# A transpose pair inside a stream of long matmuls is taken apart: one transpose before the last accumulation step, one behind it

## The reference

```
rel = pos[:, None] - pos[None, :]
mask = (rel >= 0) & (rel < 64)
attn = softmax(where(mask, q @ k.T / 8, -1e9))
x = (attn @ v), heads side by side: 2304 x 512
h = x @ w_in      # 512 x 2048
x = max(0.01 * h, h) @ w_out
h = x @ w_in2
out = (h * cos(h)) @ w_out2
```

## Time and profile before

| | |
|---|---|
| median of three runs | 912.01 us (910.81 to 912.53) |
| span of the profiled execution | 910.0 us, from the first to the last instruction |
| own time of that execution | not recorded beside its span; the median of the runs is 2.0 us above the span |
| mean granted clock of TensorE | 1.000 |
| TensorE matmuls busy | 891.0 us, 98% |
| VectorE, ScalarE, GpSimd busy | 477.5, 393.2, 83.9 us |

### The profile page before, as it was taken

How to read it: one execution, slowest core, us unless ns; L and a number is a source line. 1 busy time by engine, 2 the same in 40 slices (tenths; PEclk the granted TensorE clock), 3 DMA queues, 4 the chain that set the end, 5 groups by cost and what they waited for, 6 DMA issues and landing times.

```text
span 910.0 us, 14462 instructions
## 1 busy us (share of the span) xinstructions
PE 891.0 (98%) x5040; PEld 846.9 (93%) x5040; DVE 477.5 (52%) x1146; ACT 393.2 (43%) x978; POOL 83.9 (9%) x68
## 2 busy tenths in 40 slices
PE   6799999999999999999999999999999999999998
PEld 5799999999999999999999889998999999999997
DVE  6755555545555554555323555545545545545543
ACT  5566444433433343434345534434433434434433
POOL 2254300000000000000256400000000000000000
PEclk9999999999999999999999999999999999999999
DMA  8455322222221222220444300100200100100100
GB/s 279 136 168 177 113 77 64 64 84 63 63 71 64 76 63 73 60 67 0 142 116 139 116 1 0 69 0 0 69 0 0 69 0 0 69 0 0 36 1 36
DMA packets 36878, 59.72 MB, mean 66 GB/s; under 512 B 3952, under 2 KB 24816, under 8 KB 36848
## 3 DMA queue, kind: packets, MB, share of 16 engines
q1 hardware_dynamic: 36848, 59.33, 21.0%
HBM read 49.87 MB, written 9.44 MB: 65 GB/s over the span
## 4 chain that ended last, share of the span: by engine, by line
PE 94%; DVE 3%; ACT 1%; issue 1%; DMA 0%; SPq 0%; ACTq 0%; DVEq 0%
PE h_ps L305 43%; PE y_ps L330 22%; PE y_ps L337 21%; PE s_ps L265 3%; PE t_ps L292 3%; PE t_ps L280 1%; DVE probs L564 1%; DVE x_raw L577 1%; DMA qk_sb<-qk 0%; DVE probs L539 0%; DVE neg_max L546 0%; DVE row_sum L552 0%; ACT w_hi L400 0%; DVE act_in L598 0%; DVE probs L596 0%
## 5 line engine op out<-in xcount | busy, mean ns | idle before, releaser
L305 PE MATMUL h_ps<-x_hi,w_hi 128*128 128x384 f32 x768 | 264.0, 344 | 1.1 <-DVE g_raw L604 0.6
L305 PE MATMUL h_ps<-x_lo,w_hi 128*128 128x384 f32 x768 | 258.3, 336 | 0.0
L305 PE MATMUL h_ps<-x_hi,w_lo 128*128 128x384 f32 x768 | 257.6, 335 | 0.0
L305 PEld LDWEIGHTS h_ps<-x_hi,w_hi 128*128 128x128 f32 x768 | 144.7, 188 | 5.9 <-DVE g_raw L604 1.0
L305 PEld LDWEIGHTS h_ps<-x_hi,w_lo 128*128 128x128 f32 x768 | 144.5, 188 | 3.7
L305 PEld LDWEIGHTS h_ps<-x_lo,w_hi 128*128 128x128 f32 x768 | 144.2, 188 | 0.3 <-DVE x_lo L583 0.3
L610 DVE TENSOR_TENSOR g_lo<-g_raw,g_hi 128x384 fp32r<-128x384 f32 x192 | 107.2, 558 | 68.4 <-ACT g_hi L448 68.4
L448 ACT ACTIVATE g_hi<-g_raw 128x384 fp32r<-128x384 f32 x192 | 100.7, 524 | 93.9 <-DVE g_raw L604 56.1
L589 DVE TENSOR_TENSOR g_raw<-h_ps,act_in 128x384 f32<-128x384 f32 x96 | 53.5, 557 | 164.4 <-ACT act_in L430 164.4
L330 PE MATMUL y_ps<-g_hi,w_hi 128*128 128x384 f32 x384 | 134.1, 349 | 0.0
L430 ACT ACTIVATE act_in<-h_ps 128x384 f32<-128x384 f32 x96 | 47.1, 490 | 194.4 <-PE h_ps L305 194.4
(11 more groups left out here) (43 smaller groups left out, 961.0 us busy)
## 6 DMA issues: line engine op xcount, KB each, us to landing
qk_sb<-qk SPq DMA_DIRECT2D x72, 224.0 KB, 2.6
v_sb<-values SPq DMA_DIRECT2D x72, 128.0 KB, 2.1
w_raw<-w_in SPq DMA_DIRECT2D x32, 256.0 KB, 2.7
w_raw<-w_out SPq DMA_DIRECT2D x32, 256.0 KB, 2.9
layer_out<-y_out SPq DMA_DIRECT2D x6, 768.0 KB, 3.8
x_raw<-layer_out SPq DMA_DIRECT2D x6, 768.0 KB, 5.2
out<-y_out SPq DMA_DIRECT2D x5, 768.0 KB, 4.0
mask_sb<-mask SPq DMA_DIRECT2D x18, 128.0 KB, 2.1
```

Of the source, the lines that this page charges most:

```text
L305: mm = pe.matmul(h_ps[j % 2][:, 0:CH], w[:, j, cols], x[:, kt, :], start=kt == 0 and a == 0, stop=kt == KT - 1 and a == 2)
```

## The change

`transposes` becomes `transpose_half`, called once for each of its two blocks. The waits stay with the first half, the signal `transposed` with the second. In a tile with attention, `up` now stops ahead of its last `up_part` (kt 3); the first transpose is issued, then the three matmuls of kt 3, then the second transpose, then `down`. The loop for the first 12 units calls both halves one after the other, as before. Layer 2 and the last chunk of layer 1 have no attention, and their order is what it was.

```
+            def transpose_half(c, p, banks, a):
+
+                if a == 0:
+                    if p == 0 and banks is first_banks:
+                        pe.wait_ge(ident_in, 16)
+                    pe.wait_ge(probs_done, UNITS * c + p + 1)
+                    if banks is later_banks:
+                        pe.wait_ge(o_copied, UNITS * c + p)
+                    elif p >= 2:
+                        pe.wait_ge(probsT_done, p - 1)
+                t = banks[1][p % len(banks[1])]
+                mm = pe.transpose(t[:, P * a:P * a + P], probs[:, p % PRING, P * a:P * a + P], ident_sb[:])
+                if a == 1:
+                    mm.then_inc(transposed, 1)
+
             def transposes(c, p, banks):
...
                 for a in range(2):
-                    mm = pe.transpose(t[:, P * a:P * a + P], probs[:, p % PRING, P * a:P * a + P], ident_sb[:])
-                mm.then_inc(transposed, 1)
+                    transpose_half(c, p, banks, a)
...
-            def up(n, j):
-
-                pe.wait_ge(g_raw_done, FT * n + j - 1)
-                for kt in range(KT):
+            def up(n, j, kts=range(KT)):
+
+                if kts[0] == 0:
+                    pe.wait_ge(g_raw_done, FT * n + j - 1)
+                for kt in kts:
                     up_part(n, j, kt)
...
-                        up(*ahead)
+                        up(*ahead, range(KT - 1))
                     if attends and 1 <= j <= UNITS:
-                        transposes(n + 1, j - 1, later_banks)
+                        transpose_half(n + 1, j - 1, later_banks, 0)
+                    if not (last and j + LEAD >= FT):
+                        up(*ahead, range(KT - 1, KT))
+                    if attends and 1 <= j <= UNITS:
+                        transpose_half(n + 1, j - 1, later_banks, 1)
                     if not late:
                         down(n, j, layer)
```

More of the change, by code:

```diff
@@ L267, in scores @@
                 mm.then_inc(scores_done, 1)
-            def transposes(c, p, banks):
[L271 to L278, removed]
+            def transpose_half(c, p, banks, a):
[11 more added lines that the diff above has]
+                    mm.then_inc(transposed, 1)
+            def transposes(c, p, banks):
                 for a in range(2):
-                    mm = pe.transpose(t[:, P * a:P * a + P], probs[:, p % PRING, P * a:P * a + P], ident_sb[:])
-                mm.then_inc(transposed, 1)
+                    transpose_half(c, p, banks, a)
             def values(c, p, banks):
```

## The result

The changed kernel takes 914.03 us (median of 13 runs, 912.0 to 915.09) against 912.53 us for the kernel before (13 runs, 910.81 to 913.63): ratio 1.0018, 95% interval 1.0011 to 1.0026, that is 1.6 us more (1.0 to 2.4). The forecast was 913.9 us and 1.9 us more. That the 914.03 lies so close to 913.9 is partly luck: the kernel before came out at 912.53 in these runs and not at the 912.01 from which the forecast counted.

What follows compares the result with a forecast made beforehand. The prediction took TensorE's instruction list (matmuls busy 98%) to bound the kernel; 912.01 us plus 0.4 for pace and 1.4 for five stalls, about 1.85, gave 913.9 us, range 911.7 to 916.0.

Steps and rivals of the forecast that it cites:

- Pace: TensorE's steps around the separated transposes: two slightly longer steps into a transpose per unit, 0.4 us over 60 units.
- Rival B: TensorE's lone transposes cost only their columns, 0.06 us, saving 0.05 each, 120 times: 907.4 us; chance 6% in heading, 5% finally.
- The waits: The first transpose's waits move 0.52 us earlier; its load goes 0.11 us behind VectorE's copy; five stalls, 1.4 us.
- The cushion: At the waiting transpose on TensorE: its weight load can be 0.11 us late before the matmul is late.
- Middle units: The 50 units, 10 per chunk: the load's lead behind `copy_o` falls from 0.79 to 0.155 us, no cost.
- Rival A: The wait also bites in the 50 middle units, if a lead of 0.35 us is needed: 919.3 us; chance 6%.
- First units: First unit of five chunks: lead behind `normalise` falls from 0.60 to 0.08 us against 0.05 needed, no cost.
- Last units: Tile 12 of five chunks, lead only 0.35 us today: load 0.395 us late, matmul 0.285, 1.4 us in all.
- `up_done`'s shift: The transpose ahead of `up`'s last three matmuls delays `up_done`, and VectorE's list up to `copy_o`, by 0.115 us.
- Rival C: Stalls in tile 12 come out small, as `up_done`'s delay doesn't carry through or reaction is 0.05: 913.0 us; 18%.
- The sum: Whole kernel: 0.4 us of pace plus 1.4 us of five stalls, 1.8 to 1.9 us more, 913.9 us.
- Rival D: The 0.03 us that `down` takes longer behind a pair follows the pairing: gone, 912.1 us, 7%; doubled, 915.7 us, 5%.

Runs made afterwards that it cites:

- Experiment 3: Changed kernel, but first transpose behind `up`, second behind the first three matmuls of `down`, in all 60 units: 912.25 us against 912.0 for the kernel before.
- experiment 1: Changed kernel, but tile 12 keeps both transposes together behind `up`: 911.9 us against 912.0 for the kernel before, ratio 1.0000.
- experiment 6: Kernel before plus three identity transposes in each of 60 units: grouped behind the pair 930.25 us, single between matmuls of `down` 930.91, against 912.55.
- experiment 2: Changed kernel, but the pair is taken apart in tile 12 alone: 913.29 us against 912.0 for the kernel before, ratio 1.0012.
- experiment 4: Changed kernel, but both transposes together ahead of kt 3: 913.32 us against 912.0 for the kernel before, ratio 1.0011.

## Why the prediction was right

*Pace.* Forecast 0.4 us, bounds 0 and 0.6. Experiment 3, with all pairs apart and no stall, has 0.08 per chunk, 0.4 us; experiment 1 has 0.05. Right in size and sign for a chunk without a stall. But the few ns sit elsewhere than the sum had them. It priced one more step into a transpose at 0.007 us, read from rows rounded to 0.01. In the nanoseconds of the traces that step is 175 to 176 against 173, so 2 to 3 ns. The step behind a transpose is 108 to 109 in a pair and alone, and what is left is in the long matmuls: the two behind the lone transpose of the changed kernel take 177 each instead of 173, and the run of `down` gives a part of that back. In all, a middle tile takes 5.311 to 5.315 us and not 5.307. That the total came out at 0.4 is therefore in part luck. The Trainium skill's rule ("TensorE: Matmul & The Clock Gate", section "LDWEIGHTS (loading the stationary operand)"), 107 ns for the load of 128 columns whatever follows, agrees with these steps of 108 to 109; it says nothing of the long matmuls, and the term that is not 0 is theirs.

Rival B is refuted by experiment 6. The pull-ahead of weight loads that the Trainium skill describes (same page, section "Step-by-step: what each phase is for") shows here as one matmul and no more: in none of the eleven traces does a load start before the matmul directly ahead of it has started.

*The waits.* Needed: how long behind VectorE's copy the load goes (forecast 0.11; 0.11 to 0.12 in all five kernels with a stall or a late load), and how much lateness the matmul doesn't feel (forecast 0.11; late by 0.40, 0.29 and 0.48, lost 0.29, 0.18 and 0.37: 0.11 each time). Both came from two rows of the opening, the wait itself having never been short before. The cushion is right as a sum and not in its parts: the forecast had a transpose start 0.06 behind a late load, with 0.11 from there to the next; in the stalls it starts 0.03 behind (265.41 and 265.44), and the step behind it is 0.14 (265.44 to 265.58). The two errors of 0.03 cancel.

*Middle units.* Forecast: lead 0.155, no stall. Measured: 0.13 to 0.16, none. Rival A, for which 0.265 would have had to be needed, is out.

*First units.* Forecast 0.08 of lead for `normalise`; no stall shows there in the changed kernel, and all five idle stretches are in tile 12. Measured 0.07.

*Last units.* Forecast: load 0.395 late, 0.285 lost, 1.4 us in all. Measured 0.40, 0.29, 1.45; by the distance between the runs of `down` in tiles 11 and 12, 0.29 to 0.30 in each of the five chunks (4.86 before, 5.15 to 5.16 after).

*`up_done`'s shift.* Forecast 0.115, shown by experiments 1 and 2. In a middle unit of the changed kernel `leaky_in` starts 0.19 behind the load of `down`'s first matmul (299.31 and 299.12), before 0.09 (296.92 and 296.83). Without the shift the forecast would have been 0.6 us lower. Rival C rested on its absence, or on a reaction of 0.05, and is out.

*The sum.* Forecast 1.85. Measured 1.6 in the timed runs and 1.55 from one chunk's time. 5 x 0.29 + 0.4 is 1.85 as well. The 0.2 to 0.3 missing is in the pace: outside the stalls the changed kernel lost some 0.1 and not 0.4 us over the five chunks. In the one chunk in which no middle tile ran short it lost 0.07, which would be 0.4 for five; in each of the others one to three middle tiles took 5.29 us and not 5.31. So the term that was too large is the pace, by 0.2 to 0.3 us, and the stalls are as forecast. Rival D, in so far as it had all of the 0.03 us gone or doubled, is out.

What stays open: why some tiles run 0.02 to 0.03 shorter, and why long matmuls behind a transpose are slower.

## What to carry to other kernels

When an instruction moves forward in an engine's list, its waits move with it: for each of them read how long ahead of it the releasing work ends today, in every variant of the loop body, and take the shortest. Here ten tiles of twelve had 0.79 us of lead, the first 0.60, the last one 0.35, because it lacked one block of work; that tile alone paid. And look at what the moved instruction now delays: if the releasing work hangs on a signal that it was put in front of, the lead shrinks by its length once more. Taking small matmuls out of a group to hide them between long ones gains nothing where it is the next load that they fail to hide.

## What the runs showed of the hardware that I had not expected

- A load can come late without cost. In experiment 4 it goes 0.07 us late in a middle unit, up to 0.10 in others, and the transpose keeps its step of 0.18. Late by 0.29 to 0.48, it costs 0.11 less than it is late.
- The first five to eight long matmuls behind a transpose take up to 0.185 us and not 0.173, in a pattern that is mostly the same in every tile. Taking the pair apart left the run of `down` at 2.11 us. With the pair ahead of kt 3 it was 2.08 to 2.10, with three more transposes in front of it 2.09. Three consecutive middle tiles of experiment 4, chain in order of time:

```profile
287.65 2.10 PE y_ps L336 x12
...
292.96 2.08 PE y_ps L336 x12
...
298.26 2.09 PE y_ps L336 x12
```

  It follows the order of instructions and not ScalarE's copy of the transposes, which the change moved 0.6 us further from the first transpose (1.22 behind it, 0.58 before), with the run of `down` at 2.11 as before. Its cause was not found, and no experiment was made for it alone.
- The clock of the opening was granted at 0.92, 0.96 or 1.00 in executions of nearly the same program. Whole spans moved by more than the change did, but not with that clock: at 0.92 the first chunk's first scores load came at 37.27 in one kernel and at 39.88 in another.
